# Moving GpSimd's weight splits one place earlier in a fused attention and MLP kernel

## What is computed

```python
        C = f_stab[:, :, None, None] * C + i_stab[:, :, None, None] * np.einsum('bhd,bhe->bhde', vt, kt)
        n = f_stab[:, :, None] * n + i_stab[:, :, None] * kt
        h_tilde = np.einsum('bhde,bhe->bhd', C, qt)
        nq = np.einsum('bhd,bhd->bh', n, qt)[:, :, None]
        denom = np.maximum(np.abs(nq), 1.0)
        o = 1.0 / (1.0 + np.exp(-o_gate[:, :, t]))
        y[:, :, t] = o * h_tilde / denom
...
def _moe_ref(x, w_in, w_out, a, b):          # d_ff 2048
    h = x @ w_in
    h2 = h * h
    h3 = h2 * h
    P = a[0] + a[1] * h + a[2] * h2 + a[3] * h3
    Q = 1.0 + np.abs(b[0]) * np.abs(h) + np.abs(b[1]) * h2
    g = P / (Q + 1e-06)
    return (g @ w_out).astype(np.float32)

def _moe2_ref(x, w_gate, w_val, w_out, rms_g):   # d_ff 1536
    rms = np.sqrt(np.mean(x * x, axis=-1, keepdims=True) + 1e-06)
    xn = x / rms * rms_g
    g = xn @ w_gate
    silu = g * (1.0 / (1.0 + np.exp(-g)))
    val = xn @ w_val
    return (silu * val @ w_out).astype(np.float32)
```

## Time and profile before

| | us |
|---|---|
| median of 3 runs | 465.13 |
| lowest, highest | 464.25, 466.49 |
| the profiled execution | 463.35 |
| its span, first to last instruction | 461.3 |
| TensorE busy in the span | 453.7 |
| GpSimd busy in the span | 253.0 |

### The profile page before, as it was taken

How to read it: one execution, slowest core, us unless ns; L and a number is a source line. 1 busy time by engine, 2 the same in 40 slices (tenths; PEclk the granted TensorE clock), 3 DMA queues, 4 the chain that set the end, 5 groups by cost and what they waited for, 6 DMA issues and landing times.

```text
span 461.3 us, 7426 instructions
## 1 busy us (share of the span) xinstructions
PE 453.7 (98%) x2670; PEld 397.9 (86%) x2670; DVE 325.1 (70%) x465; ACT 289.3 (63%) x472; POOL 253.0 (55%) x274
## 2 busy tenths in 40 slices
PE   8999999989999999999999999999999999999997
PEld 4889998878999888998889888888888888888886
DVE  7998997999999999999998363474433544533333
ACT  7789887899999999999997658432122222111111
POOL 5559699879988978888899655972000000000000
PEclk9999999999999999999999999999999999999999
DMA  8999920230000000000005030000010000100001
GB/s 229 349 319 287 266 88 2 92 137 1 1 1 0 3 0 1 0 1 1 1 0 217 2 137 2 0 1 0 0 58 0 1 0 1 57 3 0 1 0 57
DMA packets 8371, 26.76 MB, mean 58 GB/s; under 512 B 1216, under 2 KB 3136, under 8 KB 7824
## 3 DMA queue, kind: packets, MB, share of 16 engines
q1 hardware_dynamic: 8336, 26.30, 18.0%
HBM read 24.33 MB, written 1.97 MB: 57 GB/s over the span
## 4 chain that ended last, share of the span: by engine, by line
PE 85%; DVE 4%; issue 1%; ACT 1%; POOL 1%; DVEq 0%; ACTq 0%; POOLq 0%
PE ps L1666 7%; PE ps L1667 7%; PE ps L1668 7%; PE ps L1596 6%; PE ps L1597 6%; PE ps L1598 6%; PE ps L1572 4%; PE ps L1614 4%; PE ps L1570 4%; PE ps L1571 4%; PE ps L1615 4%; PE ps L1616 4%; PE ps L1670 4%; PE ps L1671 3%; PE ps L1518 2%; PE ps L1573 2%
## 5 line engine op out<-in xcount | busy, mean ns | idle before, releaser
L1026 ACT ACTIVATE ab<-ps 128x512 f32<-128x512 f32 x36 | 21.6, 599 | 117.5 <-PE ps L1671 117.5
L1382 DVE TENSOR_TENSOR ab<-ps,ab 128x512 f32<-128x512 f32 x36 | 24.9, 691 | 84.3 <-ACT ab L1026 84.3
L596 POOL TENSOR_TENSOR qq<-qq,ab 128x512 f32<-128x512 f32 x48 | 61.3, 1297 | 16.9 <-ACT qq L850 16.9
L602 POOL TENSOR_TENSOR g_lo<-cc,g_hi 128x512 fp32r<-128x512 f32 x48 | 61.9, 1309 | 5.0 <-ACT g_hi L874 4.8
L1596 PE MATMUL ps<-wo_hi,g_hi 128*128 128x320 f32 x192 | 59.8, 311 | 1.3 <-DVE cc L1249 1.0
L1597 PE MATMUL ps<-wo_lo,g_hi 128*128 128x320 f32 x192 | 59.3, 309 | 0.0
L1598 PE MATMUL ps<-wo_hi,g_lo 128*128 128x320 f32 x192 | 59.3, 309 | 0.0
L1614 PE MATMUL ps<-wo_hi,g_hi 128*128 128x320 f32 x136 | 42.0, 309 | 0.2 <-ACT g_hi L1034 0.2
L1616 PE MATMUL ps<-wo_hi,g_lo 128*128 128x320 f32 x136 | 42.0, 309 | 0.0
L1615 PE MATMUL ps<-wo_lo,g_hi 128*128 128x320 f32 x136 | 42.0, 309 | 0.0
L1596 PEld LDWEIGHTS ps<-wo_hi,g_hi 128*128 128x128 f32 x192 | 36.1, 188 | 4.6 <-ACT ab L833 1.3
(11 more groups left out here) (191 smaller groups left out, 1250.5 us busy)
## 6 DMA issues: line engine op xcount, KB each, us to landing
qk<-q_k_dram SPq DMA_DIRECT2D x12, 448.0 KB, 9.3
wo_raw<-w_out_dram SPq DMA_DIRECT2D x7, 640.0 KB, 8.4
kv<-kv_n_dram SPq DMA_DIRECT2D x10, 372.0 KB, 8.0
w_raw<-w_main_dram SPq DMA_DIRECT2D x4, 512.0 KB, 8.5
out_dram<-y_out SPq DMA_DIRECT2D x12, 160.0 KB, 1.8
sig_o<-o_n_dram SPq DMA_DIRECT2D x1, 1600.0 KB, 8.5
w2c_raw<-w_main_dram SPq DMA_DIRECT2D x1, 1536.0 KB, 6.3
rest_raw<-w_rest_dram SPq DMA_DIRECT2D x2, 512.0 KB, 9.0
```

The source lines that it names most:

```text
L596: pool.tensor_tensor(qq[m % 2][:, h, :], qq[m % 2][:, h, :], ab[m % 2][:, h, :], ALU.mult)\
L602: pool.tensor_tensor(glo(n), cc[n // 2 % CR][:, n % 2, :], ghi(n).bitcast(F32), ALU.subtract)\
```

## The change

Four things. The two splits `split_main1(0)` and `(1)` come in round 3 ahead of `gated(2)`, after `decay(3)`, and no longer wait for `spread_whole(5)`. Each later split of rounds 4 to 8 comes one place sooner. After the rounds, `split_rest1(3)` comes ahead of `split_main1(5)` and of `gated(9)`. VectorE's `split_out1(0)` counts on a semaphore of its own, `out1_first`, so `low_out1(1)` no longer waits for it and `out1_ready` counts one less.

```diff
                 part = slice(2 * p, 2 * p + 2)
                 pool.wait_ge(out1_hi, p + 1)
-                pool.wait_ge(out1_ready, p)
                 pool.tensor_tensor(wo1_lo[:, part, :], wo1_raw[:, part, :], wo1_hi[:, part, :].bitcast(F32), ALU.subtract)\
                     .then_inc(out1_ready, 1)
-                pool.wait_ge(out1_ready, p + 1)
+                pool.wait_ge(out1_ready, p)
...
                 if B <= it < NT - 3:
                     decay(it)
+                if it == 3:
+                    split_main1(0)
+                    split_main1(1)
                 if it >= 1:
                     gated(it - 1)
                     normalised(it - 1)
...
-                if it == 3:
-                    pool.wait_ge(whole_spread, B + 1)
-                    split_main1(0)
-                elif it == 4:
-                    split_main1(1)
+                if it == 4:
+                    split_rest1(0)
                 elif it == 5:
-                    split_rest1(0)
-                elif it == 6:
                     split_main1(2)
                     low_out1(1)
-                elif it == 7:
+                elif it == 6:
                     split_main1(3)
                     split_rest1(1)
+                elif it == 7:
+                    low_out1(2)
+                    split_main1(4)
                 elif it == 8:
-                    low_out1(2)
+                    split_rest1(2)
                     decay(NT - 3)
-                    split_main1(4)
+                    low_out1(3)
+            split_rest1(3)
             split_main1(5)
-            split_rest1(2)
-            low_out1(3)
             gated(NT - 3)
             denominator(0)
             normalised(NT - 3)
             split_main1(6)
-            split_rest1(3)
             gated(NT - 2)
...
                 dve.wait_ge(out1_hi, p + 1)
                 dve.tensor_tensor(wo1_lo[:, part, :], wo1_raw[:, part, :], wo1_hi[:, part, :].bitcast(F32), ALU.subtract)\
-                    .then_inc(out1_ready, 1)
+                    .then_inc(out1_first, 1)
...
             def second(n):
                 j, f = divmod(n, FT1)
-                if n < FT1:
-                    pe.wait_ge(out1_ready, f // 2 + 1)
+                if n == 0:
+                    pe.wait_ge(out1_first, 1)
+                elif 2 <= n < FT1:
+                    pe.wait_ge(out1_ready, f // 2)
```

More of the change, by code:

```diff
@@ L307, in build @@
         coef_ready = sem("coef_ready")
+        out1_first = sem("out1_first")
         state_done = sem("state_done")
```

## The result

| | before | changed |
|---|---|---|
| median of 8 runs each, us | 465.01 | 468.07 |
| lowest, us | 463.25 | 466.98 |
| ratio to before, 95% interval | | 1.0077 [1.0050, 1.0104] |
| profiled execution: span, us | 461.3 | 466.7 |

The kernel became slower by 0.77%, some 3.6 us by the ratio, where +0.1 us was forecast and 463.6 to 466.8 given as the range. Without the 471.92 the means lie 3.0 us apart, 0.65%.

The account below looks back on a forecast made before the run. TensorE, busy 98% of 461.3 us, was taken as the bound. +0.44 (L1138) - 0.31 (60.07) - 0.3 (69.60) + 0 to 0.5 (pile-up) gave -0.2 to +0.3, taken as +0.1: 465.2 us, range 463.6 to 466.8.

Parts of the forecast that it names:

- L1138 late by 0.44: Round 3: split 0 holds `wv`, so `spread_whole(5)` starts at 32.70 instead of 32.26 and TensorE is 0.44 us later.
- About 1.07 us of delay per round is free: VectorE can be delayed about 1.07 us in each round before TensorE stops, as read in round 5.
- `gated(2)`, behind L1138 by up to 0.5 us, has no one waiting: Round 3: `gated(2)` may come up to 0.5 us late at no cost; its transposes come at 42 us.
- Rounds 4 to 6: Splits, each a place sooner, hold `denominators` 0.9 to 1.1 us, against 1.07 free; no loss for TensorE.
- Round 7: `low_out1(2)` and `split_main1(4)` hold `denominators(7)`; stalls of rounds 6 and 7 may pile up, costing 0 to 0.5 us.
- -0.31: Round 7: TensorE's 0.31 us wait for VectorE at 60.07 is taken up, if VectorE is no later than before.
- Round 8: `coefficients` meets a shorter split or none, so TensorE's wait up to 69.60 goes: -0.3 us.
- After 70 us: GpSimd about 1.3 us ahead with one split less before `gated(10)`; ScalarE releases both `denominator` calls, so nothing gained.
- rival 4: GpSimd is the bound after all: its 1.3 us lead passes through `denominator`, -2.3 us, 462.8; chance 0.05.
- Rival 3: Stalls of `denominators` exceed the free 1.07 us round after round as splits keep step: 3.3 us, 468.4; chance 0.06.
- rival 2: Round 3: L1138 falls behind split 1, +1.4 us less 0.6 taken up later: +0.8, 465.9; chance 0.14.

Follow-up runs that it names:

- run 5: Changed kernel with VectorE's `coefficients` moved from round 8 to behind `lo_of_x(7)`: ratio to the kernel before 1.0027, full-clock span 462.1 us.
- run 9: Changed kernel with VectorE's `coefficients` and `split_out1(0)` both moved to behind `lo_of_x(7)`: ratio to the kernel before 0.9994, full-clock span 461.6 us.
- run 10: Changed kernel with `coefficients` and `split_out1(0)` behind `lo_of_x(7)` and the pair of splits behind `ones(5)`: ratio to before 0.9968, full-clock span 460.4 us.
- run 3: Kernel before with only `split_out1(0)` counting on its own semaphore, GpSimd's order kept: ratio to the kernel before 0.9980, full-clock span 460.5 us.
- run 2: Kernel before with only the pair of splits moved in front of `gated(2)`: ratio to the kernel before 1.0015, full-clock span 461.8 us.
- run 1: Changed kernel with splits 0 and 1 put behind `ones(5)` in round 3, other moves kept: ratio to before 1.0000, full-clock span 460.9 us.
- run 7: Changed kernel with both splits in the sigmoid's wait, begun only behind `wv`: ratio to the kernel before 1.0053, full-clock span 462.6 us.
- run 6: Changed kernel with only split 0 in the sigmoid's wait, begun behind `wv`, split 1 behind `ones(5)`: ratio to before 1.0054, full-clock span 462.8 us.
- run 4: Changed kernel with five dummy matmuls in TensorE's 0.88 us wait before the transposes at 71.57: ratio to the kernel before 1.0075.

## Why the prediction was wrong

**Where the time went.** By the full-clock spans the schedule costs +2.1 us (463.2 against 461.1). The order of taking away shows its parts: `coefficients` meeting `low_out1(3)` 1.1 (run 5), `split_out1(0)` meeting `decay` and `gated` 0.5 (run 9), the pair of splits in the sigmoid's wait 1.2 (run 10); with all three away it is 0.7 better than before, about what the semaphore gives alone (0.6, run 3). The parts aren't independent: the pair alone costs 0.7 (run 2), and taking it alone away cures all 2.1 and more (run 1). Of what is left of the 3.0 to 3.6 us, the clock's dent of 1.5 us, in 5 of 7 executions instead of 16 of 79, gives some 0.8. The rest lies with the late last store (1.9 us in the profiled execution), which by the spans struck five of seven, against some 31 of 79 before, and, in the 3.6, with the run of 471.92. In all profiled executions the span ends either 2.6 to 2.7 or 4.5 to 4.9 us after the last copies; why is open, and nothing shows that the change has a part in it.

**By the steps.**

*L1138 late by 0.44*: right. `wv` took 0.90, `spread_whole` began at 32.63 with 1.22, its matmuls 0.38 later.

*"About 1.07 us of delay per round is free"*: the first failing step. It was read in round 5 and taken for every round. In round 3 `spread_whole` had already used it up, as the kernel before shows:

```profile
35.41 0.56 DVE L1237 TENSOR_TENSOR x_lo<-ps,x_hi 128x384 fp32r<-128x384 f32 x1
```

```profile
36.14 0.55 PE L1546 MATMUL ps<-ident,y 128*128 128x128 f32 x3
```

The transposes come 0.17 us behind the end of `lo_of_x`; where TensorE has to wait for it, they come 0.14 behind (36.89 and 37.03 in the changed kernel). So 0.03 us was free there, and not 1.07.

*"`gated(2)`, behind L1138 by up to 0.5 us, has no one waiting"* failed with it. No one waits for its result, but its place decides when `normalised(2)` holds the port, and that met `den`: 0.56 us more for VectorE, and TensorE 0.89 later at round 4 instead of 0.44.

*Rounds 4 to 6*: right in effect, no wait of TensorE. `wv` lost 0.8 and 1.0 in rounds 5 and 6, which I hadn't seen, since I had not asked what happens where two GpSimd instructions follow without a gap. These losses stopped no one in their own rounds, but used up what VectorE had in hand: `lo_of_x` of round 6 ended 0.14 us before its transposes, before 0.61.

*Round 7*, 0 to 0.5 for the pile-up: it was +0.36 there (1.25 against 0.89), and -0.31 did not come. `split_out1(0)` lost 1.14, within the 0.5 to 1.3 given. With the `wv` and `den` behind it VectorE lost 1.41 us in this round, before 1.52; it ended later because it had begun later.

*Round 8*, -0.3, "a shorter split or none": the step that failed by most. `decay(9)` (66.27) waited for `carry(9)`, whose matmuls on TensorE ended at 66.1, so `low_out1(3)` began at 66.97, with `coefficients`: 1.56 us for 0.17. The prediction works out no time for `decay(9)` or `low_out1(3)` and takes the kinder order. Sign and size were wrong: +0.72 instead of -0.3, a swing of 1.0. Run 5 shows it: with `coefficients` elsewhere 1.06 us go.

*After 70 us*: GpSimd's work as forecast; rival 4 fell (`denominator(0)` waited 5.47 us for ScalarE). The clock and the last store were in no term of the sum.

Rival 3, with a chance of 0.06, names the mechanism that held, den and splits keeping step round after round, but it priced only splits on `den`; `gated`, `normalised`, `decay`, `coefficients` and `wv` should have been held against the free time as well, round by round. That its 468.4 us lies near the 468.07 measured is luck: 1.4 of it was rival 2's, which did not happen, and in the measurement clock and last store stand in its place. A small misreading beside it: the gap of 0.07 us that VectorE wins is not at 46.28, where GpSimd then idles 0.72 us, but at 60.16, where the split behind it took 1.63 us for 1.28.

## What to carry to other kernels

When two engines shut each other out of a port, moving work into one engine's idle time isn't free: ask which instructions of the other run then, and also which of the *unmoved* instructions will now slide onto them in the rounds that follow. Work out the free time of each round by itself: it was 1.07 us in one and 0.03 in another. Where an engine's small extra jobs have no reader for a long time, put them where the bounding engine waits for nobody; that took the schedule's loss here from 2.1 us to 0.5 (run 9). And a wait of the matmul engine of under 1 us may cost another 1.5 in clock; count it in the range.

## What the runs showed of the hardware

- The `wv` product, with two SBUF inputs, ends 0.35 us after the GpSimd instruction that holds it; the tiny `den` (8 elements) and `coef_a` (4) end 0.02 us after.
- In a gap of 0.07 us between two GpSimd instructions VectorE gets in (`spread_whole` between the splits of run 7; the splits took 3.65 us instead of 2.77). Where they follow without a gap, it waits through both: three times in the changed kernel, where `wv` alone takes 0.49, `wv` 1.28 at 42.57, 1.48 at 48.72 and 1.20 at 61.49.
- Memsets on GpSimd did not hold `spread_whole`: 1.22 us beside them.
- TensorE's granted clock fell to 0.50 for about 3 us behind waits of 0.72 (run 6) and 0.88 us (changed), for 10 us behind one of 2.35 (run 9), and not behind waits of 0.72 (changed), 0.69 (run 4) and 0.70 (run 5), nor behind one of 0.97 to 1.01 us near 97 us in any profiled execution.
- The span ends 2.6 to 2.7 or 4.5 to 4.9 us after the last copies, from one execution to the next.
